# Attention: the second half of the key-cluster rows is made earlier in its step, in one matmul of 384 columns, with dummy matmuls in the second step

## What is computed

```
q_assign = argmax(q_n @ c_n.T); k_assign = argmax(k_n @ c_n.T)      # 16 centroids per head
mask   = q_assign[:, None] == k_assign[None, :]
scores = where(mask, q @ k.T / 8, -1e9); attn = softmax(scores)
x      = attn @ v                                                   # 16 pairs of batch and head
x      = routed_experts(x); out = dense_experts(x, gates of 8 Sinkhorn rounds)
```

## Time and profile before

| | |
|---|---|
| median of three runs | 1639.4 us |
| the profiled execution | 1642.07 us, of which 1640.3 us from the first instruction to the last |
| TensorE busy | 1591.7 us, 97% of the span |
| VectorE busy | 1198.4 us, 73% |
| ScalarE busy | 769.6 us, 47% |
| mean granted clock of TensorE | 0.991 of full speed |

### The profile page before, as it was taken

The page is one execution under the profiler, slowest core; times in us unless marked ns, Lnnn a source line. Parts: engine busy times, 40 slices in busy tenths (PEclk is TensorE's granted clock), DMA queues, the critical chain, the costliest instruction groups (busy, mean ns, idle before and its releaser), DMA issues.

```text
span 1640.3 us, 27395 instructions
## 1 busy us (share of the span) xinstructions
PE 1591.7 (97%) x8583; PEld 1410.3 (86%) x8583; DVE 1198.4 (73%) x2026; ACT 769.6 (47%) x1363; POOL 258.7 (16%) x276
## 2 busy tenths in 40 slices
PE   8999999979999989999999999999999999999998
PEld 6989998857777777899898998989989899899897
DVE  6999999989989985677566566666666656666664
ACT  4777777868888863333323323223233332332321
POOL 2111111123433341001001001000100100100102
PEclk8999999989999999999999999999999999999999
DMA  4222224053445401011001101100100100110002
GB/s 98 59 59 58 58 58 111 20 185 122 160 141 173 147 26 39 14 39 49 30 26 39 39 26 35 42 26 26 51 26 26 45 32 26 39 38 26 26 0 77
DMA packets 123699, 94.91 MB, mean 58 GB/s; under 512 B 66344, under 2 KB 101160, under 8 KB 123632
## 3 DMA queue, kind: packets, MB, share of 16 engines
q1 hardware_dynamic: 120848, 86.01, 17.5%
q0 software_dynamic: 2480, 8.13, 1.7%
q10 hardware_dynamic: 304, 0.05, 0.0%
HBM read 87.88 MB, written 6.29 MB: 57 GB/s over the span
## 4 chain that ended last, share of the span: by engine, by line
PE 89%; DVE 6%; issue 2%; ACT 2%; DMA 1%; DVEq 0%; SPq 0%; POOL 0%; ACTq 0%
PE moe_bank L1276 11%; PE moe_bank L1274 11%; PE moe_bank L1275 11%; PE moe_bank L1251 10%; PE moe_bank L1254 9%; PE moe_bank L1253 9%; PE attn_ps_probs_t L397 3%; PE attn_ps_out L416 2%; PE moe_bank L1197 2%; PE moe_bank L1199 2%; PE moe_bank L1198 2%; PE moe_bank L1210 2%; PE moe_bank L1212 2%; PE moe_bank L1211 2%; PE attn_ps_scores L386 2%
## 5 line engine op out<-in xcount | busy, mean ns | idle before, releaser
L1892 DVE SCALAR_TENSOR_TENSOR all_x<-moe_bank,all_x 128x512 f32<-128x512 f32 x336 | 251.4, 748 | 129.5 <-PE moe_bank L1276 127.3
L1251 PE MATMUL moe_bank<-moe_x_t_hi,all_w_hi 128*128 128x384 f32 x896 | 304.5, 340 | 3.0 <-DVE all_w_lo L814 2.9
L1254 PE MATMUL moe_bank<-moe_x_t_hi,all_w_lo 128*128 128x384 f32 x896 | 302.4, 338 | 0.0
L1253 PE MATMUL moe_bank<-moe_x_t_lo,all_w_hi 128*128 128x384 f32 x896 | 301.6, 337 | 0.0
L1274 PE MATMUL moe_bank<-moe_w_hi,moe_h_hi 128*128 128x512 f32 x768 | 301.1, 392 | 0.2 <-DVE moe_w_lo L814 0.2
L1275 PE MATMUL moe_bank<-moe_w_lo,moe_h_hi 128*128 128x512 f32 x768 | 300.7, 392 | 0.0
L1276 PE MATMUL moe_bank<-moe_w_hi,moe_h_lo 128*128 128x512 f32 x672 | 265.0, 394 | 0.0
L1251 PEld LDWEIGHTS moe_bank<-moe_x_t_hi,all_w_hi 128*128 128x128 f32 x896 | 168.2, 188 | 14.0 <-issue 3.6
L1253 PEld LDWEIGHTS moe_bank<-moe_x_t_lo,all_w_hi 128*128 128x128 f32 x896 | 168.2, 188 | 11.3
L1254 PEld LDWEIGHTS moe_bank<-moe_x_t_hi,all_w_lo 128*128 128x128 f32 x896 | 168.0, 187 | 0.0
L1275 PEld LDWEIGHTS moe_bank<-moe_w_lo,moe_h_hi 128*128 128x128 f32 x768 | 144.2, 188 | 22.5
(11 more groups left out here) (311 smaller groups left out, 3159.9 us busy)
## 6 DMA issues: line engine op xcount, KB each, us to landing
all_w_raw<-in_moe_w SPq DMA_DIRECT2D x8, 2048.0 KB, 7.7
moe_w_raw<-in_moe_w SPq DMA_DIRECT2D x8, 2048.0 KB, 10.0
moe_dense_w_raw<-in_moe_w SPq DMA_DIRECT2D x64, 256.0 KB, 2.9
moe_dense_w_raw<-in_moe_w SPq DMA_DIRECT2D x32, 512.0 KB, 3.3
attn_q_raw<-in_q SPq DMA_DIRECT2D x32, 192.0 KB, 3.4
attn_k_raw<-in_k SPq DMA_DIRECT2D x32, 192.0 KB, 3.8
attn_v_raw<-in_v SPq DMA_DIRECT2D x16, 192.0 KB, 3.8
tokens<-all_x SPq DMA_DIRECT2D x32, 96.0 KB, 2.0
```

The lines of the kernel that those rows point to most:

```text
L1251: pe.matmul(out, hi[:, s, k, :], XH[chunk][:, x, k, :], start=(start and k == 0), stop=False, skip_group_check=True)
L1253: pe.matmul(out, hi[:, s, k, :], XL[chunk][:, x, k, :], start=False, stop=False, skip_group_check=True)
L1254: mm = pe.matmul(out, lo[:, s, k, :], XH[chunk][:, x, k, :], start=False, stop=(stop and k == 1), skip_group_check=True)
L1892: dve.scalar_tensor_tensor(acc, y, PROB[:, row, bass.ds(at, 1)], acc, ALU.mult, ALU.add).then_inc(y_added, 1)
```

## The change

Three edits. The call of stage 6 is taken out of the loop over the stages at the end of a step and placed behind the transposes of the probabilities on TensorE, and behind the two copies of `evacuate` on ScalarE. `key_ids` makes its 384 columns with one matmul in place of three of 128. And in the second step of the program (i = 0, s = 1) TensorE issues six matmuls of ones into ps_out, ahead of stage 5. In the constants and in TensorE's function:

```diff
-WARM = (8, 4)
+WARM = (8, 4, 6)
...
             def key_ids(out, first):
-                for n in range(first, first + 3):
-                    mm = pe.matmul(out[:, (n - first) * P:(n - first + 1) * P], c["onesb"][:], DIAG[:, n, :],
-                                   start=True, stop=True)
-                mm.then_inc(prep_ready, 1)
+                pe.matmul(out[:, 0:3 * P], c["onesb"][:], DIAG[:, first:first + 3, :].rearrange("p n k -> p (n k)"),
+                          start=True, stop=True).then_inc(prep_ready, 1)
...
             def step(i, s):
                 n = 12 * i + s
                 transpose_probs(n, s)
+                prep_ahead(i, s, (6,))
                 if s % 3 == 2 and any_before(i, s):
                     fold(i, s)
...
-                for head, stage in ahead(s):
-                    if not isinstance(i, int) or 2 * i + head < G:
-                        prep(2 * i + head, head % 2, stage, i + head // 2)
+                if isinstance(i, int) and i == 0 and s == 1:
+                    pe.wait_ge(x_done, 1)
+                    warm(WARM[2], ps_o[:])
+                prep_ahead(i, s, (0, 1, 2, 3, 4, 5))
```

More of the change, by code:

```diff
@@ L442, in step, with prep_ahead, warm @@
                     values(s % 3, i, s)
-                for head, stage in ahead(s):
-                    if not isinstance(i, int) or 2 * i + head < G:
-                        prep(2 * i + head, head % 2, stage, i + head // 2)
+                if isinstance(i, int) and i == 0 and s == 1:
+                    pe.wait_ge(x_done, 1)
+                    warm(WARM[2], ps_o[:])
+                prep_ahead(i, s, (0, 1, 2, 3, 4, 5))
                 if s % T == 0 and any_before(i, s):
                     values(s % 3, i, s)
-            def warm(n):
+            def prep_ahead(i, s, stages):
+                for head, stage in ahead(s):
+                    if stage in stages and (not isinstance(i, int) or 2 * i + head < G):
+                        prep(2 * i + head, head % 2, stage, i + head // 2)
+            def warm(n, out=ps_s[0][:, 0, :]):
                 ones = c["onesb"][:].rearrange("p (o k) -> p o k", o=1).broadcast_to([P, 4, P])
                 for _ in range(n):
-                    pe.matmul(ps_s[0][:, 0, :].rearrange("p (o k) -> p o k", o=4), c["onesb"][:], ones, start=True, stop=True)
+                    pe.matmul(out.rearrange("p (o k) -> p o k", o=4), c["onesb"][:], ones, start=True, stop=True)
             pe.wait_ge(made, 3)
```

## The result

The changed kernel takes 1633.67 us (median of five, 1631.69 to 1635.26), the kernel before 1639.82 (median of five, 1639.2 to 1642.11): a ratio of 0.9955, 95% interval 0.9944 to 0.9966, 0.45% faster. The profiled execution of the changed kernel is the slowest of its five, 1635.26 us with a span of 1633.5.

The account below looks back on a forecast made before the run. The prediction took each head as a ring with TensorE and VectorE both nearly full, gaining the smaller of what they can give up. First head 3.1 plus 13 x 0.50 = 6.5, together 9.6: 1642.07 to 1632.5 us, range 1629.5 to 1636.1.

Parts of the forecast that it names:

- The sum: Whole kernel: first head 3.1 us plus thirteen heads at 0.50 each, 6.5, together 9.6 off 1642.07, giving 1632.5 us.
- VectorE's 0.50: VectorE's waits behind the masks of stage 0 (0.34 too much) and stage 1 (0.16) vanish: 0.50 us a head.
- TensorE's larger number: TensorE can give up 0.66 us a head; as the pace-setter this was a rival, 1630.6 us, chance 0.14.
- the 0.59 of the wait itself: Stage 0's raw transposes (L331) wait for ScalarE's copy of the second half of the key rows (L518), 0.59 us each.
- TensorE's side: Stage 6 moved ahead of the fold: raw transposes start at 93.45 against 94.11, so TensorE gives up 0.66 us a head.
- The slack behind the scores: VectorE's maximum starts about 0.35 us after the scores end; the moved key matmul uses 0.17 of it.
- One matmul for three: Key matmul of 384 columns for three of 128: no gain taken; the skill page's price would save 2.2 us.
- ScalarE: Copy goes ahead of exponentials, which begin 0.5 us later; it waits for nothing; about 0.15 us margin before the raw copy.
- The dummies: Six matmuls in the second step take 1.3 us, keep the clock full behind them; at half clock, stage 5 slips 0.8 us.
- The 2.26 us for a low stretch: From raw transposes to L604, head 0 takes 9.70 us and head 1, at full clock, 7.44: low clock costs 2.26.
- The spread of the runs: The low clock in the second step, 2.26 us, accounts for runs of 1639.2 and 1639.4 against 1642.11.
- moves as a block: What follows attention (last steps, routing, expert layers) hangs on its end and shifts with it; nothing is lost there.

## Why the prediction came out right

- **The sum.** Forecast 1632.5 us, measured 1633.67 and, in a later run, 1632.78. Thirteen heads were to take 248.4 us: 248.5. The step that carried it was to ask what each engine could give up, and to take VectorE's 0.50 and not TensorE's larger number or the 0.59 of the wait itself. The runs with more work for TensorE and less for VectorE show that this was the cause.
- **Luck in it.** The 0.50 is right for the steady heads (19.60 to 19.11). The second head gains 0.55, the third only 0.19, the fourth 0.37, and the last two, which were longer before (19.82 and 19.70), gain 0.71 and 0.60. That these make up for each other was not forecast.
- **TensorE's side** was mis-sized: I had 0.66 us to give and TensorE at L340 at 101.7 beside VectorE's 101.95, a spare of some 0.26; it is 0.34 by the run with six more transposes, and 0.55 - 0.18 = 0.37 by the starts. The raw transposes start without the 0.10 for a wait in the loop: counted from the cluster search at 91.79 - 85.49 = 6.30 in place of 94.11 - 87.05 = 7.06, 0.76 us earlier. It changed nothing, since the other engine set the pace.
- **The slack behind the scores** was wrong. "VectorE's maximum starts about 0.35 us after the scores end; 0.17 of it is used": the 0.35 us were counted from the end of the key matmuls (93.52). VectorE's maximum before, behind the scores that end at 93.00 + 0.34 = 93.34, in its timeline:

```profile
93.87 0.96 DVE L640 CUSTOM_DVE_ANT_0 attn_scores<-attn_ps_scores,attn_mask 128x768 f32<-128x768 f32 x1
```

That is 0.53 us after them. It starts at best 0.41 after, and the three-matmul run shows it following the scores. The slack was about 0.12, less than the 0.17, and it is used up. It cost little here, 0.04 us in a steady head (6.85 where the outputs' reading at 6.50 would have let it start at 6.81).
- **One matmul for three**: I took nothing, by the spacing of the matmuls within their group. It is 0.08 us on TensorE and, through the maximum, 0.06 a head, some 0.8 us in thirteen heads. The price lay behind the group, where I had not looked.
- **ScalarE** did as forecast: the exponentials later ((91.21 - 85.49) - (92.39 - 87.05) = 0.38 us, not 0.5, counted from the search), no wait for the key matmul, a margin of 0.19 ahead of the raw copy.
- **The dummies.** In the first head I forecast 3.1 us, 21.55 down to 18.45; with a full clock it is 18.39. But the profiled execution had the clock low where I had it full, and took 19.75. The 2.26 us for a low stretch was right for the kernel before (2.4); that the stretch also moves about ahead of the dummies, and makes them cost, I had named only as a bound. Over the runs they are worth 0.3 and 1.6 us in the changed kernel and 1.4 in the kernel before, with overlapping intervals; a gain of that size is likely, not shown.
- **The spread of the runs** I put down to the low clock in the second step alone. The profiles show more places: the stretch ahead of it (above), and the part behind the last search, which takes 1336.6 to 1340.3 us in the fourteen profiles. That this part is equal within 0.4 us in the two profiles of the forecast, and so "moves as a block", is luck in part.
- Not settled: the third head of every kernel that has the move on both engines is 0.2 to 0.3 us longer than its later ones, the fourth of most by 0.1, and those before the change were not. In the third head of the changed kernel the fold starts 0.28 us behind the moved key matmul, where it is 0.17 in the steady heads, and takes 0.88 in place of 0.79; the scores come 0.24 us later and VectorE's maximum behind them 0.25 (7.10 from the search against 6.85). What holds the fold up wasn't tried.

## What to carry to other kernels

When two engines run in a ring, a wait that is removed is worth the smaller of what the two can give up: count for each engine the pauses that the removal closes, and take the smaller sum. Afterwards look for the wait on the other engine that has grown (here L340, from 0.10 to 0.37 us); adding work to one engine and taking some from the other shows in two runs which of them is the bound, for the part of the ring in which the work stands. An operation moved away from a collision can meet the next one: look at every place where the loop runs, the first steps too. Read the price of a group of small matmuls from the start of the work two instructions behind it, not from the spacing within.

## What the hardware showed that I had not expected

- Half-clock stretches between 8 and 38 us come at different places in different executions: 11 to 18 and 31 to 38 us in one, 12.5 to 19 and 22.2 to 33 in another, about 13.5 to 16.5 alone in three. The one that began at 22.2 came while TensorE was busy all the time, from 19.7 to 21.6 with small matmuls (16 columns, 8 rows).
- The runs of one kernel differ by 0.5 to 6 us. The part behind the last search varies by 3.7 us, more than the part ahead of the first search (2.3 us), and the granted clock with it: it is 1340.3 us in the three-matmul profile, where the mean clock is 0.73 from 325 to 350 us and 0.67 from 610 to 620, and 1336.6 in the one with six more transposes, where it is 0.86 and 1.00.
- VectorE's maximum starts 0.41 or 0.42 us after the end of the last score matmul in fifteen places of the changed kernel's profile, and never sooner after one; three waits, each with a semaphore increment, stand ahead of the instruction. The cluster search, which has one wait, starts 0.03 or 0.04 us after the end of L344. That the waits are what costs the difference wasn't tried.
- A tiny operation of VectorE (128 x 3) takes 0.47 us in place of 0.15 when it meets a cast of GpSimd, and a mask 0.85 in place of 0.42 beside GpSimd's diagonal, or 1.01 beside a subtraction of GpSimd's of 1.00 us; the subtraction from PSUM is not slowed.
